# Constant products on TensorE in the long waits of both routings

## What is computed

```python
def _moe_ref(x, w_skip, w_gate, w1, w2):          # N, D, E, F = 3072, 512, 8, 1024
    do_compute = x @ w_skip > 0
    xc = x[do_compute]
    logits = xc @ w_gate
    e_idx = np.argmax(logits, axis=1)
    ...
    for e in range(E):
        mask = e_idx == e
        y[mask] = gate_w[mask, None] * (np.maximum(xc[mask] @ w1[e], 0.0) @ w2[e])
    out[do_compute] = xc + y

def _moe2_ref(x, w_gate, w1, w2):
    cap = N // E
    order = np.argsort(-(x @ w_gate).flatten())
    for idx in order:
        tok, e = (int(idx) // E, int(idx) % E)
        if assigned[tok] >= 0 or counts[e] >= cap:
            continue
        assigned[tok] = e
        counts[e] += 1
    for e in range(E):
        mask = assigned == e
        out[mask] = np.maximum(x[mask] @ w1[e], 0.0) @ w2[e]
```

## Time and profile before

| | us |
|---|---|
| median of 3 runs | 919.61 |
| the runs | 926.02, 919.61, 914.32 |
| the profiled execution | 920.52 |
| its span, first to last instruction | 918.8 |
| PE busy | 769.8 |
| DVE busy | 388.0 |
| ACT busy | 220.5 |
| POOL busy | 185.6 |
| mean granted clock of TensorE | 0.92 |

### The profile page before, as it was taken

One profiled execution on the slowest core, in us unless ns is written; L12 is line 12 of the kernel. 1 busy time (PEld: TensorE's weight loads), 2 busy tenths in 40 slices (PEclk: granted clock), 3 DMA queues, 4 the chain that ended last, 5 costly groups with the idle time before them and its releaser, 6 DMA issues.

```text
span 918.8 us, 14353 instructions
## 1 busy us (share of the span) xinstructions
PE 769.8 (84%) x4727; PEld 524.7 (57%) x4727; DVE 388.0 (42%) x1530; ACT 220.5 (24%) x685; POOL 185.6 (20%) x236
## 2 busy tenths in 40 slices
PE   2788888877079999994329999999999999999995
PEld 1788888877057777682225454454545545555552
DVE  4585767845602121113763636346363553620000
ACT  2666667754001111010001011110111101111110
POOL 4472736323021111111010020111101011031101
PEclk8898999989579999997558999999999999999998
DMA  8999795999073518600050330504205050155000
GB/s 187 201 244 227 183 244 129 244 254 293 13 280 130 194 58 322 246 7 7 1 218 1 126 127 1 218 34 164 88 10 208 35 218 35 53 220 197 35 0 34
DMA packets 137827, 126.02 MB, mean 137 GB/s; under 512 B 100722, under 2 KB 100722, under 8 KB 137584
## 3 DMA queue, kind: packets, MB, share of 16 engines
q1 hardware_dynamic: 125584, 94.74, 34.1%
q10 hardware_dynamic: 6432, 14.73, 5.6%
q0 software_dynamic: 5760, 15.87, 4.6%
HBM read 105.80 MB, written 22.74 MB: 140 GB/s over the span
## 4 chain that ended last, share of the span: by engine, by line
PE 66%; DVE 10%; DMA 9%; issue 5%; POOL 5%; SPq 2%; ACT 1%; POOLq 1%; DVEq 0%; ACTq 0%
PE bank L1085 19%; PE bank L1098 13%; PE bank L978 8%; PE bank L993 8%; DMA scratch<-rows_b,idx 4%; PE bank L1026 3%; DMA weights<-in_k 3%; PE bank L868 3%; PE bank L847 2%; POOL weights L626 2%; PE bank L1046 1%; PE bank L1058 1%; PE bank L857 1%; POOL scratch L657 1%; PE bank L890 1%
## 5 line engine op out<-in xcount | busy, mean ns | idle before, releaser
L1085 PE MATMUL bank<-scratch,weights 128*128 128x384 f32 x512 | 183.6, 503 | 0.7 <-ACT scratch L1261 0.7
L1098 PE MATMUL bank<-weights,scratch 128*128 128x512 f32 x384 | 178.8, 610 | 5.0 <-issue 2.5
L1085 PEld LDWEIGHTS bank<-scratch,weights 128*128 128x128 f32 x512 | 94.2, 192 | 59.7 <-issue 5.8
L1098 PEld LDWEIGHTS bank<-weights,scratch 128*128 128x128 f32 x384 | 70.3, 193 | 79.2 <-issue 76.4
L1167 ACT ACTIVATE scratch<-shared,neg_max 128x120 f32<-128x120 f32 x192 | 73.4, 383 | 45.6 <-DVE neg_max L1316 30.9
L1267 ACT ACTIVATE scratch<-bank 128x384 f32<-128x384 f32 x64 | 31.4, 490 | 171.1 <-PE bank L1085 171.1
L657 POOL TENSOR_TENSOR scratch<-scratch,row_inv 128x480 f32<-128x480 f32 x48 | 47.3, 986 | 99.2 <-DVE row_inv L1326 98.5
L978 PEld LDWEIGHTS bank<-mix,weights 128*128 128x128 f32 x512 | 60.6, 196 | 4.6 <-issue 4.6
L978 PE MATMUL bank<-mix,weights 128*128 128x128 f32 x512 | 61.5, 279 | 0.9 <-DVE mix L1522 0.9
L868 PE MATMUL bank<-shared,mix 120*128 120x128 f32 x384 | 53.2, 283 | 6.3 <-issue 6.3
L993 PE MATMUL bank<-weights,mix 128*128 128x512 f32 x128 | 58.4, 599 | 0.0
(11 more groups left out here) (234 smaller groups left out, 971.0 us busy)
## 6 DMA issues: line engine op xcount, KB each, us to landing
weights<-in_moe_w SPq DMA_DIRECT2D x20, 2048.0 KB, 11.6
scratch<-in_moe_w SPq DMA_DIRECT2D x8, 2048.0 KB, 15.6
weights<-in_moe_w ACTq DMA_DIRECT2D x16, 512.0 KB, 6.6
mix<-in_v SPq DMA_DIRECT2D x40, 192.0 KB
rows_a<-row SPq DMA_DIRECT2D x24, 260.5 KB, 4.1
rows_b<-row SPq DMA_DIRECT2D x24, 260.0 KB, 4.4
weights<-in_k SPq DMA_DIRECT2D x24, 256.0 KB, 5.6
scratch<-in_q SPq DMA_DIRECT2D x24, 256.0 KB, 4.8
```

What stands on the lines that cost most here:

```text
L1085: last = mm(hb2[f % 2][:, 0:CAP], w1_sb[odd][:, c, f * P:(f + 1) * P], xT2[odd][:, c, :], start=(c == 0), stop=(c == C - 1), skip_group_ch ...
L1098: last = mm(yb2[c % 2][:, :], hT2[odd][:, f, c * P:(c + 1) * P], w2_sb[odd][:, f, :], start=(f == 0), stop=(f == FC - 1), skip_group_check ...
```

## The change

A function `idle_products(n)` issues n products of the constant matrix with itself into the first 128 columns of bank 4. Nobody reads them. It is called before waits of both routings: 75, 160 and 130 times in the first, and in the second with a number for each step. Each call issues n weight loads of 128 x 128 bf16 and n products of 128 columns. A wait for `consts_pool`, which other engines raise in the first microseconds, stands ahead of the first call.

```diff
             ranks, sums, table = bank[0], bank[1], bank[2]
 
+            def idle_products(n):
+
+                for _ in range(n):
+                    mm(bank[4][:, 0:P], before[:, :], before[:, :], start=True, stop=True)
+
+            pe.wait_ge(s.consts_pool, CONSTS + 1)
+            idle_products(75)
             pe.wait_ge(s.phase_ready, 1)
             mm(ranks[:, 0:NT * E], before[:, :], chosen_h.rearrange("p j e -> p (j e)"), start=True, stop=True)
             mm(sums[:, 0:NT * E], ones[:, :], chosen_h.rearrange("p j e -> p (j e)"), start=True,
                stop=True).then_inc(s.ranked_ps, 1)
+            idle_products(160)
             pe.wait_ge(s.phase_ready, 2)
...
+            idle_products(130)
             pe.wait_ge(s.gathered, 16)
             turn1()
...
+            pauses = {0: 130, 2 * ROUNDS: 26, 2 * ROUNDS + 1: 20, 2 * ROUNDS + 2: 24, 2 * ROUNDS + 3: 28}
             for n in range(STEPS):
+                idle_products(pauses.get(n, 17 if n % 2 == 0 else 0))
                 step(0, n)
             for n in range(AHEAD):
+                idle_products((36, 0, 17, 0)[n])
                 step(1, n)
+            idle_products(28)
             turn2(0, 0)
```

## The result

The changed kernel takes 923.46 us (median of 9 runs, 918.83 to 925.38), the kernel before 916.36 (9 runs beside it, 911.19 to 926.02): a ratio of 1.0067, with 95% interval 1.0036 to 1.0099. So it is slower, but by less than the 2% within which the prediction speaks of the same time. The profiled execution is one of 925.38 us with a span of 923.6.

The account below looks back on a forecast made before the run. It took PE's half clock in the two routings, where PE waits on DVE and the gather, as the cost. +2.9 us in the first and -5.2 in the second gave -2.3 on 920.5: 918 us, range 910 to 928.

Parts of the forecast that it names:

- Does it hold?: Second routing: bursts make PE busy some 2.0 in 3.4 us, narrowly enough to keep the clock up; counted on, not firmly.
- Price of a product: Each added product with its load costs 0.057 us at full clock and 0.11 at half.
- Rival C: Both routings: each product costs 0.117 us whatever the clock, so +16 us, or 937; chance 0.10.
- First routing: Third burst of 130 ends 5.3 us late; 2.25 and 0.15 come back, net +2.9 us.
- Rival D: First routing: third burst at full clock or products nearer 0.038, late by 3 us or less; 916 us; chance 0.12.
- Second routing: Clock holds through counts, transposes and first up products of the second experts: -5.2 us in sum.
- First up products: Second experts: 5.54 us of up products at half clock would run at full clock, gaining 2.7 us.
- Counts: Second routing: full clock saves 1.4 us over four rounds of 63-column counts, 0.1 for all small ones.
- Transposes: Before the second experts: 12 transposes with their copies go from 3.58 to some 2.6 us, gaining 1.0.
- To the first count: Second routing: 130 products take 9.6 us in 10.16 us of cover, hidden by a hair, so no cost.
- To the second transposes: Second routing's end: no cost charged; bursts of 36 and 28 may bring the clock back before the experts.
- rival B: Second routing: clock down again for the second experts' first products, losing 3.2 us of gain; 921.4 us; chance 0.30.

Follow-up runs that it names:

- after again: The changed kernel run once more on the first chip, against the kernel before: 917.2 us, ratio 1.001.
- fitted: Changed kernel with bursts cut to their waits (40 for the third 130, 12 for the last 28, others resized), against before: 916.4 us, ratio 0.9967.
- second_again: Kernel before plus the second routing's bursts alone, repeated as a control: 917.38 us in one run, beside before at 917.4.
- second_shift: Kernel before plus the second routing's bursts and 59 products in the first routing's first wait, shifting later instructions: 914.61 us in one run, before 917.4.
- before again: The unchanged kernel before, run once more on the second chip for another profile: 919.18 us, ratio 1.0.

## Why the prediction was wrong, point by point

The forecast was 918.0, 1.6 below the median shown, by -2.3 on the profiled execution; the kernel is 6.1 us slower by the ratio (3.3 to 9.1 by its interval), and 0.9 and 2.6 in the two repeats. The sign of the forecast was wrong in all three, though only the first interval leaves out 1. What failed is the step "Does it hold?", that the clock stays up through the second routing, and with it two costs there that the prediction put at nothing.

**Price of a product: right.** 75 in 4.35 us and 130 in 7.42 are 0.058 and 0.057 us each at full clock; 28 in 3.17 at half are 0.113. I had 0.057 and 0.11. Rival C (0.117, +16 us) fell at once. The Trainium skill, TensorE: Matmul & The Clock Gate, section "Wait — 56ns, not 53.3ns?", has about 62 ns for each MATMUL without hardware decode. Rows of 75 and 130 at 57 to 58 ns, load included, lie below it; whether the chip decoded in hardware here no run shows.

**First routing: right.** The burst starts 29.84 us after the attention's end in after; with 224.46 that is the 254.3 of the forecast. It took 9.24 us for 9.6, made the transposes 4.87 us late for 5.3, and 2.16 came back for 2.25: +2.7 of +2.9. The other profiles with the 130 have 17.75, 17.70 and 17.28 us in that stage, against 17.86 in after; those with none there have 12.84 to 13.07. Rival D, with the transposes on time, is out.

**Second routing: the step that failed.** I had -5.2; the profile has -1.4. Term by term:

- First up products: -2.7 forecast, -2.73 measured. The other two profiles of the changed kernel have 3.42 too. But before has it by itself in one of three profiles (3.42 in the first repeat, 6.15 and 6.32 in the others), so on the average less of it, some 1.9 us by these three, is the change's to give.
- Counts: -1.5 forecast, -0.33 measured. This is "Does it hold?". I set 2.0 busy us in 3.4 on the side where the clock stays; it fell twice in the counts. The changed kernel's other profiles have 32.43 and 31.69, so -0.3 to -1.1 by execution. With 30 products for 17 it held in three profiles of four, and gave the 1.2.
- Transposes: -1.0 forecast, -0.19 measured. They ran at half, 2.71 us for 2.91; the clock had fallen at 479.05, while PE waited 2.02 us for the late signal, and the 17 and 28 behind it did not bring it back. The prediction had named the 36 and 28 as what might. Where the clock came back among them, in after again and without the third burst, the stage was 2.96 us, 0.6 less than before.
- To the first count: nothing forecast, +0.62, the instruction fetch. The prediction charged the products' time and not their code.
- To the second transposes: nothing forecast, +1.24. The burst of 28 took 3.17 us at half clock and the first count of list 1 had come late by the signal, so that together they outlasted the gather. With signals on time and the same 3.17 the stage is 12.58 and 12.59 (after again and without the third burst, first chip); with the late signal, on the third chip, it is 14.31 in both kernels, and 12.60 where the bursts are 10 and 12 (`fitted`). So the overrun needs both, the late signal and the long bursts. The bursts were changed by themselves; the signal was not, and its part is argued from the pairing.

Half of rival B happened: the clock was down in the thin waits and at the transposes, but back for the up products. By the rule of the same page of the Trainium skill, section "Part 4: PE-mode transpose", the full clock does not engage for transposes; the profile of before again disagrees, where 3.40 us with 2.91 of transposes and nothing else on PE end with the clock raised.

**The sum.** The terms as measured give +2.7 - 1.4 = +1.2 us in the touched stages; the other two profiles of the changed kernel have 264.51 and 265.41 there, and before has 262.41 and 265.19 beside its 265.50: means of 265.6 and 264.4, again +1.2, though three profiles that scatter by 3 us cannot tell that from nothing. The three comparisons of runs have 1.0067, 1.001 and 1.0028, or +6.1, +0.9 and +2.6 us. I can account for 1.2 with places; the rest of the first comparison's 6.1 is not placed, lies in its profile in stages with no changed instruction, and stays open. The late signal may be in it: the changed kernel stood worst where its profile has late signals (+6.1 and +2.6) and best where it has none (+0.9), and the 1.7 us that it costs at the second transposes are hidden in before. What is shown by removal is the third burst, which costs 3.4 and 4.6 us between medians; its +2.7 in the stages lies within their uncertainty. Without it the rest of the change gains 0.3%: 0.9966 and 0.9967. No kernel compared over 12 runs goes beyond that.

## What to carry to other kernels

Filling a wait to keep the clock pays only if the burst ends before the wait does at the clock that it will really have: count from when the engine is free (here after nine register loads), at the half-clock price, and leave room for a late landing; 40 products did in 3.96 us what 130 did too late. A filler in a thin wait has to keep the clock up to earn anything, and at half clock it can itself hold up the work behind it. Its code is fetched by DMA too, and such a fetch lengthened short transfers here. What waited with room to spare before may have none once the wait is filled: a delay that before hid cost the changed kernel 1.7 us. Read the gain of a raised clock over several profiles of the kernel before, since the edge of the clock may already lie ahead of the work in some.

## What the runs showed of the hardware

- A 16 KB instruction fetch early in a DMA of small pieces lengthened it from 3.67 to 4.39 us (`second_again` against `second_shift`, 4.30 in after); 2.8 us into it, a fetch did not (3.71). An indirect one with a fetch in it took 3.04 to 3.77 us for 2.25 (three profiles). Which transfer was hit changed with the number of instructions ahead.
- On the second and third chip DVE went on 0.9 to 1.8 us late behind a count of PE that ended while POOL issued an indirect DMA, or up to 0.2 us before; on the first and fourth it was never more than 0.4 us late. What holds it up was not shown.
- The clock came back at the end of a stretch where PE did nothing but 12 f32 transposes, 2.91 of 3.40 us (before again, 478.80 to 482.20).
- Long rows of product and load of 128 bf16 columns each kept 0.057 to 0.058 us a pair at full clock, and DVE's large comparisons beside them took 943 ns, as in before.
- Where the clock falls and rises moved between executions of one kernel: the same up products took 3.42, 6.15 and 6.32 us in three profiles of before.
